# Retention, a softplus feed-forward layer and top-1 experts on one core: loading the first three chunks at once

## The chip, the cores and the metric

The kernel runs on one core of a Trainium2 chip. Its engines work side by side and meet only at semaphores: TensorE multiplies matrices, VectorE and ScalarE work element by element, GpSimd does the same more slowly, and SyncE issues the DMAs (each engine issues its own instructions strictly in order). The metric is the time of one execution on the device in microseconds (us), lower is better.

## The reference

What has to be computed, cut to what matters (4 batches, 8 heads, 768 positions, head size 64; all inputs and outputs are float32):

```python
# stage 1: decayed linear attention, one state per batch and head
for t in range(S):
    state = gamma * state + einsum('bhd,bhe->bhde', k[:, :, t], v[:, :, t])
    y[:, :, t] = scale * einsum('bhd,bhde->bhe', q[:, :, t], state)
x = y.transpose(0, 2, 1, 3).reshape(3072, 512)
# stage 2: dense feed-forward, 512 -> 2048 -> 512
h = x @ w_in
x = (maximum(h, 0) + log1p(exp(-abs(h)))) @ w_out          # softplus
# stage 3: each token goes through the one of 8 experts that its gate picks, 512 -> 1024 -> 512
e = argmax(x @ w_gate, axis=1)
out = softmax_weight_of_e * (maximum(x @ w1[e], 0) @ w2[e])
```

## The kernel before, in words

**Stage 1 by chunks.** The recurrence is cut into chunks of 128 positions, six for each batch. A chunk needs four loads of 256 KB: kT, qT, k and v. `heads` (TensorE, L1156) makes the scores of the eight heads from kT and qT; `masked` (VectorE, L724, twice) multiplies them by the table `decay` into two buffers of probabilities; on GpSimd, `decays` multiplies q by `qdec` (L449) and k by `kdec` (L451); `attend_to` (TensorE) adds up the values under the probabilities (L1171), updates the running state in PSUM (L1178) and, from the second chunk on, adds the part that comes from the state before (L1184). The state that it reads is made by `read_state` (VectorE, L731). The chunk's result goes to `XS` as a rounded high part (`x_high`, ScalarE, L547) and the rest as a low part (`x_low`, VectorE, L739), because stage 2 multiplies in a format that keeps fewer bits: three products (high·high, high·low, low·high) stand for one.

**Stage 2 by blocks and strips.** Three chunks make a block of 384 tokens; there are eight blocks. A block runs through 16 strips of the 2048 hidden columns. `strip_h` (TensorE, L1205, 12 matmuls) makes a strip of h; ScalarE computes the softplus in three passes (L578, L580, L582) and rounds it (`strip_high`, L562); VectorE finishes it (`strip`, L763) and takes the low part (`strip_low`, L767); `strip_out` (TensorE, L1220, 9 matmuls) multiplies it by w_out. TensorE runs `strip_h(g)` two strips ahead of `strip_out(g - 2)`. The attention of the next block is laid between the strips: in the turn of g = 2, 7 and 12 the `heads` of one chunk stands right behind `strip_h(g)` (list `A1_AT`), and `attend_to` in the turns 4, 9 and 14 (`A2_AT`). In the first block these are chunks 3, 4 and 5.

**The dense weights.** w_in and w_out (4 MB each) come in eight pieces of 1 MB, w_in and w_out in turn, through three staging buffers `raw[0..2]`. Each piece is rounded into `W` by `piece_high` (ScalarE, L552), and `piece_low` (VectorE, L745) writes the low part and so frees the staging buffer. Pieces 0, 1 and 2 are split while the first three chunks are computed, pieces 3 to 7 during the first block, in the strips that `PIECES_AT` lists. `strip_h(g)` needs piece 2(g/4), `strip_out(g)` piece 2(g/4) + 1, for g = 0, 4, 8 and 12.

**The queue of loads.** All these loads are issued by SyncE in one written order, and it waits, in order, until the buffer of each is free. In the first block the order is: chunk 3, pieces 3 to 7, the small `gate_k`, chunk 4, `w_gate` (2 MB, its buffer lies where the staging was, so it waits until the last piece is split), chunk 5. A chunk has one set of load buffers, so chunk c + 1 is loaded when chunk c has left them.

**The start.** `load_chunk(0, 0)` brings chunk 0 and the tables (`decay` 512 KB, `qdec` 256 KB, the small table 164.5 KB), and then for each chunk its loads and one piece follow each other. TensorE goes through `heads` and `attend_to` chunk by chunk, in PSUM banks given by `START_AT`. Nothing of stage 2 can start before x_low of chunk 2.

Stage 3 (routing, gathers, expert weights) is not touched.

Of the kernel before, what the change touches and what calls it, by code (L numbers as in the profile page):

```python
# [68 lines left out]
PIECES_AT = [1, 3, 4, 6, 7]  # L69
# [34 lines left out]
def build(nc, qT, kT, k, v, w_in, w_out, w_gate, w_gate_k, w1, w2, table, out):  # L104
    x_rows = nc.dram_tensor("x_rows", [NTOK, D], F32, kind="Internal").ap()

    with ExitStack() as ctx:
# [223 lines left out]
        def _(sp):  # L331
            def load_chunk(b, c6):
                c = b * CB + c6
                first = isinstance(c, int) and c == 0
                src = slice(c6 * D, (c6 + 1) * D)
                if not first:
                    sp.wait_ge(s_qk if isinstance(c, int) and c <= SUB else s_att, c)
                sp.dma_start(kT_c, kT[b_at(b), :, src].rearrange("o p n -> (o p) n")).then_inc(s_kT, 16)
                if not first:
                    sp.wait_ge(s_qd, c)  # L340
                sp.dma_start(qT_c, qT[b_at(b), :, src].rearrange("o p n -> (o p) n")).then_inc(s_qT, 16)
                if first:
# [26 lines left out]
            load_chunk(0, 3)  # L369
            for n in range(3, 2 * NPIECE):  # L370
                load_piece(n)
# [33 lines left out]
            def one(i, half, attend, first):  # L405
# [5 lines left out]
                if first:  # L411
                    sp.wait_ge(s_wlo, 2 * NPIECE)
# [30 lines left out]
        def _(pool):  # L443
            def decays(b, c6):
                c = b * CB + c6
                pool.wait_ge(s_qT, 16 * (c + 1))
                if not (isinstance(c, int) and c == 0):
                    pool.wait_ge(s_att, c)
                pool.tensor_tensor(qd, qT_c, qdec, ALU.mult).then_inc(s_qd, 1)  # L449
                pool.wait_ge(s_k, 16 * (c + 1))  # L450
                pool.tensor_tensor(blk(k_c, H), blk(k_c, H), kdec[:, c6, :].unsqueeze(2).broadcast_to([P, H, HD]),  # L451
                                   ALU.mult).then_inc(s_kd, 1)

            pool.wait_ge(s_tab, 32)
            for c6 in range(SUB):
                decays(0, c6)
# [83 lines left out]
        def _(act):  # L540
# [8 lines left out]
            def piece_high(n):  # L549
                act.wait_ge(s_raw[n % 3], 16 * (n // 3 + 1))  # L550
# [3 lines left out]
            for c6 in range(SUB):  # L554
                x_high(0, c6, START_AT[c6])
                piece_high(c6)
# [41 lines left out]
            def shifted(i, half, attend, first=False):  # L598

                m = 2 * i + half  # L600
                for g in range(1, GF + 1):
# [4 lines left out]
                    if first and g in PIECES_AT:  # L606
                        piece_high(3 + PIECES_AT.index(g))
# [106 lines left out]
        def _(dve):  # L714
# [27 lines left out]
            def piece_low(n):  # L742
                dve.wait_ge(s_whi, n + 1)
# [3 lines left out]

            for c6 in range(SUB):
# [196 lines left out]
            def shifted(i, half, attend, first):  # L945
                m = 2 * i + half
                for g in range(1, GF + 1):
# [8 lines left out]
                    if first and g in PIECES_AT:  # L956
                        piece_low(3 + PIECES_AT.index(g))
# [186 lines left out]
        def _(pe):  # L1144
            def heads(b, c6, at=0):
# [3 lines left out]
                pe.wait_ge(s_kT, 16 * (c + 1))  # L1149
                pe.wait_ge(s_qT, 16 * (c + 1))  # L1150
                if at == 0 and not (isinstance(c, int) and c == 0):
                    pe.wait_ge(s_xlo, 1 if isinstance(c, int) and c < SUB else c)
                for h in range(H):
                    rows = slice((h % 2) * HD, (h % 2 + 1) * HD)
                    cols = slice((h // 2) * P, (h // 2 + 1) * P)
                    last = pe.matmul(ps[:, at + h % 2, cols], kT_c[rows, cols], qT_c[rows, cols],  # L1156
                                     start=True, stop=True)
                last.then_inc(s_qk, 1)

            def attend_to(b, c6, at=0):  # L1160
                c = b * CB + c6
                pe.wait_ge(s_v, 16 * (c + 1))
# [6 lines left out]
                for h in (0, 2, 1, 3, 4, 6, 5, 7):  # L1169
                    bank, out_rows, out_cols = spot(h)  # L1170
                    last = pe.matmul(ps[out_rows, at + bank, out_cols], v_c[:, h * HD:(h + 1) * HD],  # L1171
                                     probs_of(h % 2, c)[:, (h // 2) * P:(h // 2 + 1) * P], start=(h < 4),
                                     stop=True, skip_group_check=True)
                if c6 < CB - 1:
                    for h in range(H):
                        rows = slice((h % 2) * HD, (h % 2 + 1) * HD)
                        head = slice(h * HD, (h + 1) * HD)
                        last = pe.matmul(blk(ps_s, PAIRS)[rows, h // 2, :], k_c[:, head], v_c[:, head],  # L1178
                                         start=(c6 == 0 and h < 2), stop=True, skip_group_check=True)
                if c6:  # L1180
                    for h in range(H):
# [277 lines left out]
```

## Time and profile before

| quantity | value |
|---|---|
| runs | 1039.24, 1039.69, 1042.95 us; median 1039.69 us |
| profiled execution | 1037.87 us, span 1036.1 us |
| mean granted TensorE clock | 0.987 of full speed |
| TensorE busy | 993.4 us, 96% of the span |
| VectorE / ScalarE / GpSimd busy | 507.7 / 430.3 / 164.3 us (49%, 42%, 16%) |
| chain that ended last | TensorE 90%, VectorE 2%, DMA 2%, "issue" 2%, ScalarE 1%, GpSimd 1% |

How to read it: the span runs from the first to the last instruction of the profile; the profiled execution's own time is 1.8 us longer. TensorE is busy in nine tenths or more of each slice except the first and the last; in the first of the 40 slices (26 us each) it is busy for four tenths and in the second for seven. The page and the answers of the trace name an instruction by its line in the kernel and by the tensors that it writes and reads; `arena` is the big shared buffer in which most small tiles lie. "SPq" rows are DMA issues of SyncE. Rows of L1171, L1156, L1178 and L1184 count two records for each matmul.

### The profile page before, as it was taken

The page shows a single profiled execution, that of the slowest core. Times are in us where ns is not written, and L with a number is a line of the kernel's source. Part 1 is how long each engine was busy: PE and PEld are TensorE (multiplying, and loading weights), DVE is VectorE, ACT ScalarE, POOL GpSimd, SP SyncE. Part 2 cuts the span into 40 slices and gives each one's busy share as a digit, 9 for nine tenths or more (in the row PEclk, how much of TensorE's full clock was granted, in tenths as well). Part 3 has the DMA queues.
Part 4 walks back from the last instruction along what each step waited for, and adds up shares of the span by engine and source line. Part 5 has one row for each costly group of instructions (what it writes and reads, how often), then busy time and mean ns, then how long its engine had stood idle before and what let it go on. Part 6 is the DMA issues. An engine that isn't in the chain of part 4 may idle for free.

```text
span 1036.1 us, 18904 instructions
## 1 busy us (share of the span) xinstructions
PE 993.4 (96%) x5968; PEld 859.0 (83%) x5969; DVE 507.7 (49%) x997; ACT 430.3 (42%) x754; POOL 164.3 (16%) x172
## 2 busy tenths in 40 slices
PE   4799999999999999999999999999999999999994
PEld 4688888888788888888888898787888888888783
DVE  2563265455465465456456487555222422445552
ACT  1473543533443443444444546424223323435451
POOL 2200010111111111111111000221111312232230
PEclk8799999999999999999999999999999999999998
DMA  6633121121121121121121013237111311552570
GB/s 220 251 105 114 41 72 42 41 72 42 43 71 42 41 72 41 43 71 42 41 72 41 31 41 122 73 122 274 53 40 40 114 40 40 193 205 73 189 261 15
DMA packets 28631, 91.89 MB, mean 89 GB/s; under 512 B 4046, under 2 KB 4174, under 8 KB 23312
## 3 DMA queue, kind: packets, MB, share of 16 engines
q1 hardware_dynamic: 23760, 76.48, 21.2%
q0 software_dynamic: 4800, 14.42, 4.3%
q8 instruction: 50, 0.82, 0.3%
q14 instruction: 21, 0.17, 0.1%
HBM read 78.30 MB, written 13.89 MB: 89 GB/s over the span
## 4 chain that ended last, share of the span: by engine, by line
PE 90%; DVE 2%; issue 2%; DMA 2%; ACT 1%; DVEq 1%; POOL 1%; ACTq 0%; SPq 0%; POOLq 0%
PE ps L1205 25%; PE ps L1220 25%; PE ps L1334 15%; PE ps L1309 14%; PE ps L1171 3%; PE ps L1156 2%; PE ps L1319 2%; PE ps L1184 1%; PE ps L1293 1%; PE ps L1178 1%; POOL arena L451 1%; DMA arena<-k 1%; DMA small_tab<-table 1%; DVE W L987 1%; DMA arena<-x_rows,arena 1%
## 5 line engine op out<-in xcount | busy, mean ns | idle before, releaser
L1205 PE MATMUL ps<-XS,W 128*128 128x384 f32 x1536 | 292.0, 338 | 4.8 <-issue 2.2
L1220 PE MATMUL ps<-W,GS 128*128 128x512 f32 x1152 | 292.1, 398 | 2.2 <-DVE GS L767 2.2
L1205 PEld LDWEIGHTS ps<-XS,W 128*128 128x128 f32 x1536 | 273.6, 189 | 17.6 <-issue 2.8
L1220 PEld LDWEIGHTS ps<-W,GS 128*128 128x128 f32 x1152 | 211.3, 188 | 48.4 <-DVE GS L767 3.3
L1334 PE MATMUL ps<-W,XS 128*128 (+1 forms) x696 | 167.3, 396 | 4.5 <-DVE XS L997 4.5
L1309 PE MATMUL ps<-W,XS 128*128 (+1 forms) x696 | 170.6, 394 | 0.0
L578 ACT ACTIVATE arena<-ps 128x384 f32<-128x384 f32 x128 | 62.8, 491 | 232.1 <-PE ps L1205 228.6
L1334 PEld LDWEIGHTS ps<-W,XS 128*128 128x128 f32 x696 | 129.7, 190 | 31.6 <-issue 5.6
L1309 PEld LDWEIGHTS ps<-W,XS 128*128 128x128 f32 x696 | 128.4, 188 | 25.5 <-DVE XS L991 0.3
L763 DVE SCALAR_TENSOR_TENSOR arena<-ps,arena 128x384 f32<-128x384 f32 x128 | 71.1, 555 | 135.0 <-ACT arena L582 135.0
L778 DVE CUSTOM_DVE_ANT_0 arena<-arena 128x512 bf16<-128x512 f32 x168 | 128.3, 802 | 0.0
L449 POOL TENSOR_TENSOR arena<-arena 128x512 f32<-128x512 f32 x24 | 37.6, 1567 | 465.9 <-DMA arena<-qT 445.4
L649 ACT ACTIVATE XS<-ps 128x512 fp32r<-128x512 f32 x58 | 31.5, 595 | 171.3 <-PE ps L1319 155.4
L767 DVE TENSOR_TENSOR GS<-arena,GS 128x384 fp32r<-128x384 f32 x128 | 75.0, 586 | 0.1
L997 DVE TENSOR_TENSOR XS<-ps,XS 128x512 fp32r<-128x512 f32 x58 | 37.4, 686 | 76.4 <-ACT XS L649 41.9
L582 ACT ACTIVATE arena<-arena 128x384 f32<-128x384 f32 x128 | 67.2, 525 | 4.0
L580 ACT ACTIVATE arena<-arena 128x384 f32<-128x384 f32 x128 | 67.2, 525 | 4.0
L987 DVE TENSOR_TENSOR W<-arena,W 128x2048 f32 (+1 forms) x28 | 62.8, 2286 | 9.6 <-ACT W L630 9.6
L739 DVE TENSOR_TENSOR XS<-ps,XS 128x512 fp32r<-128x512 f32 x24 | 16.6, 692 | 100.6 <-ACT XS L547 100.6
L562 ACT ACTIVATE GS<-arena 128x384 fp32r<-128x384 f32 x128 | 65.0, 508 | 0.5 <-DVE arena L763 0.5
L547 ACT ACTIVATE XS<-ps 128x512 fp32r<-128x512 f32 x24 | 14.4, 598 | 113.1 <-PE ps L1184 89.7
L1004 DVE TENSOR_SCALAR arena<-ps,arena 128x512 f32<-128x512 f32 x28 | 20.9, 748 | 81.5 <-PE ps L1334 81.5
(160 smaller groups left out, 675.7 us busy)
## 6 DMA issues: line engine op xcount, KB each, us to landing
arena<-w SPq DMA_DIRECT2D x32, 1024.0 KB, 7.0
arena<-kT SPq DMA_DIRECT2D x24, 256.0 KB, 2.7
arena<-qT SPq DMA_DIRECT2D x24, 256.0 KB, 2.9
arena<-v SPq DMA_DIRECT2D x24, 256.0 KB, 4.1
arena<-k SPq DMA_DIRECT2D x24, 256.0 KB, 4.2
x_rows<-arena SPq DMA_DIRECT2D x24, 256.0 KB, 4.5
arena<-w_in SPq DMA_DIRECT2D x4, 1024.0 KB, 6.8
arena<-w_out SPq DMA_DIRECT2D x4, 1024.0 KB, 7.7
```

The source lines that it names most:

```text
L562: act.activation(GS[:, par, 0, :], soft[par], ACT.Copy).then_inc(s_ghi, 1)
L578: act.activation(soft[par], ps_h[par], ACT.Abs).then_inc(s_abs, 1)
L580: act.activation(soft[par], soft[par], ACT.Exp, scale=-1.0).then_inc(s_exp, 1)
L582: act.activation(soft[par], soft[par], ACT.Ln, bias=1.0).then_inc(s_ln, 1)
L763: dve.scalar_tensor_tensor(soft[par], ps_h[par], 0.0, soft[par], ALU.max, ALU.add).then_inc(s_g, 1)
L767: dve.tensor_tensor(GS[:, par, 1, :], soft[par], GS[:, par, 0, :].bitcast(F32), ALU.subtract).then_inc(s_glo, 1)
L778: dve.tensor_tensor_reduce(out=junk[e % 2], in0=x_out[s], in1=gate_w[:, e * D:(e + 1) * D], scale=1.0, scalar=0.0, op0=ALU.mult, op1=ALU.a ...
L987: dve.tensor_tensor(dst, raw_w[:, cols], hi, ALU.subtract).then_inc(s_out, 1)
L1205: last = pe.matmul(ps_h[g % 2], w_in_s[a][:, g // 4, k_, (g % 4) * P:(g % 4 + 1) * P], xs[half][b][:, k_, :], start=(k_ == 0 and a + b == ...
L1220: last = pe.matmul(ps_x[s], GS[:, g % 2, a, s * P:(s + 1) * P], w_out_s[b][:, g, :], start=(g == 0 and a + b == 0), stop=(g == GF - 1 and ...
L1309: last = pe.matmul(ps_h1[n], tx[a][:, k_ * P:(k_ + 1) * P], w, start=(k_ == 0 and a + b == 0), stop=(k_ == KD - 1 and a == 1))
L1334: last = pe.matmul(ps_y2, th[a][:, k_ * P:(k_ + 1) * P], w, start=(k_ == 0 and a + b == 0), stop=(k_ == GE - 1 and a == 1))
```

## The change

- The first three chunks have buffers of their own: chunk 0 those of before, chunks 1 and 2 four quarters each of `raw[1]` and `raw[2]`. Their loads are issued without a wait, chunk after chunk (`load_first`), with `qdec` moved behind the first two loads of chunk 1. Chunk 3 is issued behind them and behind piece 0.
- Each load has a semaphore that is waited for where its data is used. GpSimd no longer decays q of chunk 0 (nothing reads it), and decays k before q; q of chunk 2 goes to a buffer of its own.
- TensorE issues `heads` of chunk 1 ahead of the attention of chunk 0, and waits for the decayed k only ahead of the state update (`first_attend`). VectorE reads the state after the masks, and takes x_low of a chunk one chunk later.
- Piece 0 comes and is split in two halves. Since `raw[1]` and `raw[2]` hold chunks, pieces 1 and 2 are loaded when chunks 1 and 2 are done. Before the first strip, pieces 0 and 1 are split; pieces 2 to 7 are split in strips 1, 3, 5, 7, 9 and 11 of the first block. Before, pieces 3 to 7 were split in strips 1, 3, 4, 6 and 7.
- `low_done(n)` is the count that says that piece n is split, now with one more for the halves.

```diff
-PIECES_AT = [1, 3, 4, 6, 7]
+PIECES_AT = [1, 3, 5, 7, 9, 11]
...
+        s_qdec = sem("q_decay_loaded")
         s_kT, s_qT, s_k, s_v = sem("kT_loaded"), sem("qT_loaded"), sem("k_loaded"), sem("v_loaded")
         s_raw = [sem(f"raw_loaded{i}") for i in range(3)]
+        s_raw0 = [sem(f"first_raw_half{i}") for i in range(2)]
+        s_qk_in, s_kv_in = ([sem(f"{w}_loaded{c}") for c in (1, 2)] for w in ("qT_kT", "k_v"))
...
+        def loaded(c):
+            return 16 * (c - 1)
+        def chunk(c, i):
+            return raw[c][:, i * D:(i + 1) * D] if isinstance(c, int) and 0 < c < SUB else (kT_c, qT_c, k_c, v_c)[i]
+        def qd_of(c):
+            return start_odd if isinstance(c, int) and c == SUB - 1 else qd
         def probs_of(half, c):
-            return probs_even if half == 0 else start_odd if isinstance(c, int) and c < SUB else kT_c
+            return probs_even if half == 0 else start_odd if isinstance(c, int) and c == 0 else chunk(c, 0)
+        def low_done(n):
+            return n + 2
...
+            def load_first(c):
+                src, rows = slice(c * D, (c + 1) * D), slice(c * P, (c + 1) * P)
+                sp.dma_start(chunk(c, 0), kT[0, :, src]).then_inc(s_qk_in[c - 1] if c else s_kT, 16)
+                sp.dma_start(chunk(c, 1), qT[0, :, src]).then_inc(s_qk_in[c - 1] if c else s_qT, 16)
+                if c == 0:
+                    sp.dma_start(decay, table[:, T_DECAY:T_QDEC]).then_inc(s_dec, 16)
+                if c == 1:
+                    sp.dma_start(qdec, table[:, T_QDEC:T_KDEC]).then_inc(s_qdec, 16)
+                sp.dma_start(chunk(c, 3), v[0, rows, :]).then_inc(s_kv_in[c - 1] if c else s_v, 16)
+                if c == 0:
+                    sp.dma_start(small_tab[:], table[:, T_KDEC:T_COLS]).then_inc(s_tab, 16)
+                sp.dma_start(chunk(c, 2), k[0, rows, :]).then_inc(s_kv_in[c - 1] if c else s_k, 16)
             def load_chunk(b, c6):
                 c = b * CB + c6
-                first = isinstance(c, int) and c == 0
                 src = slice(c6 * D, (c6 + 1) * D)
-                if not first:
-                    sp.wait_ge(s_qk if isinstance(c, int) and c <= SUB else s_att, c)
+                sp.wait_ge(s_qk if isinstance(c, int) and c == SUB else s_att, 1 if isinstance(c, int) and c == SUB else c)
                 sp.dma_start(kT_c, kT[b_at(b), :, src].rearrange("o p n -> (o p) n")).then_inc(s_kT, 16)
-                if not first:
+                if not (isinstance(c, int) and c == SUB):
                     sp.wait_ge(s_qd, c)
                 sp.dma_start(qT_c, qT[b_at(b), :, src].rearrange("o p n -> (o p) n")).then_inc(s_qT, 16)
-                if first:
-                    sp.dma_start(decay, table[:, T_DECAY:T_QDEC]).then_inc(s_dec, 16)
+                if isinstance(c, int) and c == SUB:
+                    sp.wait_ge(s_att, 1)
                 else:
                     sp.wait_ge(s_att, c)
                     sp.wait_ge(s_kd, c)
                 rows = slice(c6 * P, (c6 + 1) * P)
                 sp.dma_start(v_c, v[b_at(b), rows, :].rearrange("o p n -> (o p) n")).then_inc(s_v, 16)
-                if first:
-                    sp.dma_start(qdec, table[:, T_QDEC:T_KDEC]).then_inc(s_tab, 16)
-                    sp.dma_start(small_tab[:], table[:, T_KDEC:T_COLS]).then_inc(s_tab, 16)
                 sp.dma_start(k_c, k[b_at(b), rows, :].rearrange("o p n -> (o p) n")).then_inc(s_k, 16)
             def b_at(b):
                 return bass.ds(b, 1)
             def load_piece(n):
-                if n >= 3:
-                    sp.wait_ge(s_wlo, n - 2)
+                if n < 3:
+                    sp.wait_ge(s_att, n + 1)
+                else:
+                    sp.wait_ge(s_wlo, low_done(n - 3))
                 src = w_in if n % 2 == 0 else w_out
                 sp.dma_start(raw[n % 3], src[:, (n // 2) * PIECE:(n // 2 + 1) * PIECE]).then_inc(s_raw[n % 3], 16)
-            load_chunk(0, 0)
-            load_piece(0)
-            load_chunk(0, 1)
-            load_piece(1)
-            load_chunk(0, 2)
-            load_piece(2)
-            load_chunk(0, 3)
-            for n in range(3, 2 * NPIECE):
+            for c in range(SUB):
+                load_first(c)
+            for i in range(2):
+                cols = slice(i * PIECE // 2, (i + 1) * PIECE // 2)
+                sp.dma_start(raw[0][:, cols], w_in[:, cols]).then_inc(s_raw0[i], 16)
+            load_chunk(0, SUB)
+            for n in range(1, 2 * NPIECE):
...
-                    sp.wait_ge(s_wlo, 2 * NPIECE)
+                    sp.wait_ge(s_wlo, low_done(2 * NPIECE - 1))
...
+            pool.wait_ge(s_tab, 16)
+            pool.wait_ge(s_k, 16)
+            decay_k(0, 0)
+            pool.sem_inc(s_qd, 1)
+            pool.wait_ge(s_qdec, 16)
+            for c in range(1, SUB):
+                pool.wait_ge(s_kv_in[c - 1], 32)
+                decay_k(c, c)
+                pool.wait_ge(s_qk_in[c - 1], 32)
+                if c == SUB - 1:
+                    pool.wait_ge(s_att, 1)
+                pool.tensor_tensor(qd_of(c), chunk(c, 1), qdec, ALU.mult).then_inc(s_qd, 1)
...
+            def first_piece_high(i):
+                act.wait_ge(s_raw0[i], 16)
+                cols = slice(i * PIECE // 2, (i + 1) * PIECE // 2)
+                act.activation(W[:, 0, 0, cols], raw[0][:, cols], ACT.Copy).then_inc(s_whi, 1)
+            x_high(0, 0, START_AT[0])
+            x_high(0, 1, START_AT[1])
+            first_piece_high(0)
+            first_piece_high(1)
+            x_high(0, 2, START_AT[2])
+            piece_high(1)
...
-                        piece_high(3 + PIECES_AT.index(g))
+                        piece_high(2 + PIECES_AT.index(g))
...
             for c6 in range(SUB):
                 if c6 == 1:
-                    dve.wait_ge(s_tab, 32)
-                if c6:
-                    read_state(0, c6)
+                    dve.wait_ge(s_tab, 16)
                 masked(0, c6, 0, START_AT[c6])
                 masked(0, c6, 1, START_AT[c6])
                 if c6:
-                    piece_low(c6 - 1)
-                x_low(0, c6, START_AT[c6])
-            piece_low(SUB - 1)
+                    read_state(0, c6)
+                    x_low(0, c6 - 1, START_AT[c6 - 1])
+            first_piece_low(0)
+            first_piece_low(1)
+            x_low(0, SUB - 1, START_AT[SUB - 1])
+            piece_low(1)
...
-                        piece_low(3 + PIECES_AT.index(g))
+                        piece_low(2 + PIECES_AT.index(g))
...
+            def first_attend(c, at):
+                if c:
+                    pe.wait_ge(s_kv_in[c - 1], 32)
+                else:
+                    pe.wait_ge(s_v, 16)
+                pe.wait_ge(s_probs, 2 * c + 2)
+                values(c, at)
+                pe.wait_ge(s_kd, c + 1)
+                if c:
+                    pe.wait_ge(s_state, c)
+                    pe.wait_ge(s_qd, c + 1)
+                last = update(c, c)
+                if c:
+                    last = from_state(c, at)
+                last.then_inc(s_att, 1)
+            heads(0, 0, START_AT[0])
+            heads(0, 1, START_AT[1])
+            first_attend(0, START_AT[0])
+            first_attend(1, START_AT[1])
+            heads(0, 2, START_AT[2])
+            first_attend(2, START_AT[2])
...
-                    pe.wait_ge(s_wlo, 2 * (g // 4) + 1)
+                    pe.wait_ge(s_wlo, low_done(2 * (g // 4)) if g else 1)
...
+                    if isinstance(n, int) and n == 0 and k_ == KD // 2:
+                        pe.wait_ge(s_wlo, 2)
```

TensorE at the start of the program, before. L1156 is `heads`, L1171 the values, L1178 the state update, L1184 the part from the state.

```order
L1156 MATMUL ps<-arena 128x128 [waits qT_loaded,kT_loaded]
L1156 MATMUL ps<-arena 128x128 x7
L1171 MATMUL ps<-arena 64x128 [waits probs_ready,k_decayed,v_loaded]
L1171 MATMUL ps<-arena 64x128 x7
L1178 MATMUL ps<-arena 64x64 x8
L1156 MATMUL ps<-arena 128x128 [waits qT_loaded,kT_loaded]
L1156 MATMUL ps<-arena 128x128 x7
L1171 MATMUL ps<-arena 64x128 [waits k_decayed,state_ready,probs_ready,q_decayed,v_loaded]
```

The same place in the changed kernel, where these are L1214, L1222, L1231 and L1239.

```order
L1214 MATMUL ps<-arena 128x128 [waits qT_loaded,kT_loaded]
L1214 MATMUL ps<-arena 128x128 x7
L1214 MATMUL ps<-arena 128x128 [waits qT_kT_loaded1]
L1214 MATMUL ps<-arena 128x128 x7
L1222 MATMUL ps<-arena 64x128 [waits probs_ready,v_loaded]
L1222 MATMUL ps<-arena 64x128 x7
L1231 MATMUL ps<-arena 64x64 [waits k_decayed]
L1231 MATMUL ps<-arena 64x64 x7
L1222 MATMUL ps<-arena 64x128 [waits probs_ready,k_v_loaded1]
L1222 MATMUL ps<-arena 64x128 x7
L1231 MATMUL ps<-arena 64x64 [waits q_decayed,state_ready,k_decayed]
```

The second chunk's scores now stand ahead of the first chunk's values, and the values no longer wait for the decayed k.

VectorE at the last piece of the dense weights, before: L745 is `piece_low(7)`, in strip 7. The mask behind it (L724) is the second one of chunk 4.

```order
L731 TENSOR_TENSOR arena<-ps,small_tab 128x256 [waits attention_done]
L724 TENSOR_TENSOR arena<-ps,arena 128x512 [waits attention_done,scores_ready]
L763 SCALAR_TENSOR_TENSOR arena<-ps,arena 128x384 [waits ln_done]
L767 TENSOR_TENSOR GS<-arena,GS 128x384 [waits softplus_high]
L745 TENSOR_TENSOR W<-arena,W 128x2048 [waits dense_high]
L724 TENSOR_TENSOR arena<-ps,arena 128x512 [waits attention_done,scores_ready]
```

The last piece in the changed kernel: L793 is `piece_low(7)`, in strip 11. L818 and L822 are a strip's two operations, L779 and L772 behind it the state and the first mask of chunk 5.

```order
L818 SCALAR_TENSOR_TENSOR arena<-ps,arena 128x384 [waits ln_done]
L822 TENSOR_TENSOR GS<-arena,GS 128x384 [waits softplus_high]
L793 TENSOR_TENSOR W<-arena,W 128x2048 [waits dense_high]
L779 TENSOR_TENSOR arena<-ps,small_tab 128x256 [waits attention_done]
L772 TENSOR_TENSOR arena<-ps,arena 128x512 [waits attention_done,scores_ready]
```

The last split moved from between the two masks of chunk 4 to right ahead of the masks of chunk 5.

SyncE in the first block of the changed kernel: the last piece, `gate_k`, chunk 4 (L368 to L379), `w_gate`, and chunk 5's first loads. The order before is the same.

```order
L390 DMA arena<-w_out 128x2048 [waits dense_low]
L400 DMA gate_k<-w_gate_k 128x32
L368 DMA arena<-kT 128x512 [waits attention_done]
L371 DMA arena<-qT 128x512 [waits q_decayed]
L378 DMA arena<-v 128x512 [waits k_decayed,attention_done]
L379 DMA arena<-k 128x512
L441 DMA arena<-w_gate 128x4096 [waits dense_low]
L368 DMA arena<-kT 128x512 [waits attention_done]
L371 DMA arena<-qT 128x512 [waits q_decayed]
```

No row moved here; piece 7 still waits for piece 4's split and `w_gate` for piece 7's, and these splits stand in other strips now.

## Rows read from the trace of the kernel before

**Rows 1.** Chain of waits, first 60 us; start, length (us), what ran or was awaited.
```profile
3.09 6.08 DMA small_tab<-table
...
14.83 3.03 DMA arena<-k
...
17.92 2.73 POOL arena L451
...
20.90 1.98 PE ps L1171 x16
...
23.73 1.11 PE ps L1184 x16
...
36.54 3.82 PE ps L1205 x12
...
54.95 1.02 PE ps L1171 x16
```

**Rows 2.** Chain of waits from 36 us to 130 us, one warm strip.
```profile
83.80 2.10 PE ps L1205 x12
```

**Rows 3.** Busy time by windows; last three columns granted clock, DMA share, GB/s.
```profile
8.00:10.00 2.00, 0.00 (x0) 0.00 (x0) 0.77 (x2) 0.00 (x0) 0.76 (x1) 1.00 0.99 407
```

**Rows 4.** Timeline of all engines, one early chunk; start, length, what, idle before.
```profile
24.73 1.79 PE L1156 MATMUL ps<-arena 64*128 64x128 f32 x16
24.86 0.60 ACT L547 ACTIVATE XS<-ps 128x512 fp32r<-128x512 f32 x1 [8.00 <-PE ps L1184]
...
25.36 1.90 ACT L552 ACTIVATE W<-arena 128x2048 fp32r<-128x2048 f32 x1
25.49 0.69 DVE L739 TENSOR_TENSOR XS<-ps,XS 128x512 fp32r<-128x512 f32 x1 [5.75 <-ACT XS L547]
...
26.10 0.41 DVE L731 TENSOR_TENSOR arena<-ps,small_tab 128x256 f32<-128x256 f32 x1
...
26.56 1.29 DVE L724 TENSOR_TENSOR arena<-ps,arena 128x512 f32<-128x512 f32 x2
...
27.77 2.28 DVE L745 TENSOR_TENSOR W<-arena,W 128x2048 fp32r<-128x2048 f32 x1
```

**Rows 5.** Busy time by windows again, granted clock third from last.
```profile
26.00:26.50 0.50, 0.50 (x8) 0.32 (x6) 0.50 (x2) 0.50 (x1) 0.26 (x1) 0.92 0.45 53
...
29.50:30.00 0.50, 0.00 (x0) 0.00 (x0) 0.50 (x1) 0.00 (x0) 0.50 (x1) 0.50 1.00 410
...
39.50:40.00 0.50, 0.50 (x3) 0.50 (x3) 0.39 (x1) 0.00 (x0) 0.50 (x1) 0.77 0.65 262
```

**Rows 6.** Timeline around piece 7 and chunk 4 in the first block.
```profile
56.74 0.33 SPq L361 DMA_DIRECT2D arena<-w_out  x1
...
58.07 0.43 SPq L341 DMA_DIRECT2D arena<-qT  x1
...
62.96 0.51 ACT L562 ACTIVATE GS<-arena 128x384 fp32r<-128x384 f32 x1
...
69.72 1.16 PE L1156 MATMUL ps<-arena 64*128 64x128 f32 x16
```

**Rows 7.** DMA issues in 58.05 to 58.4 us: KB, us to landing.
```profile
arena<-qT SPq DMA_DIRECT2D x1, 256.0 KB, 6.1
```

**Rows 8.** Timeline around w_gate and chunk 5.
```profile
76.01 0.33 SPq L413 DMA_DIRECT2D arena<-w_gate  x1
...
81.97 0.42 SPq L341 DMA_DIRECT2D arena<-qT  x1
...
91.64 0.51 ACT L562 ACTIVATE GS<-arena 128x384 fp32r<-128x384 f32 x1
...
94.21 1.16 PE L1156 MATMUL ps<-arena 64*128 64x128 f32 x16
```

**Rows 9.** DMA issues at 76.01 and 81.97 us: KB, us to landing.
```profile
arena<-w_gate SPq DMA_DIRECT2D x1, 2048.0 KB, 8.1
...
arena<-qT SPq DMA_DIRECT2D x1, 256.0 KB, 3.5
```

More of the change, by code:

```diff
@@ L443, in _, with decay_k @@
         def _(pool):
+            def decay_k(c, c6):
+                pool.tensor_tensor(blk(chunk(c, 2), H), blk(chunk(c, 2), H),
+                                   kdec[:, c6, :].unsqueeze(2).broadcast_to([P, H, HD]), ALU.mult).then_inc(s_kd, 1)
             def decays(b, c6):
                 c = b * CB + c6
-                pool.wait_ge(s_qT, 16 * (c + 1))
-                if not (isinstance(c, int) and c == 0):
-                    pool.wait_ge(s_att, c)
+                pool.wait_ge(s_qT, loaded(c))
+                pool.wait_ge(s_att, c)
                 pool.tensor_tensor(qd, qT_c, qdec, ALU.mult).then_inc(s_qd, 1)
[L450 to L456, printed above, removed]
+                pool.wait_ge(s_k, loaded(c))
+                decay_k(c, c6)
+            pool.wait_ge(s_tab, 16)
[10 more added lines that the diff above has]
+                pool.tensor_tensor(qd_of(c), chunk(c, 1), qdec, ALU.mult).then_inc(s_qd, 1)
             def one(i, half, attend, first):
@@ L742, in piece_low @@
             def piece_low(n):
-                dve.wait_ge(s_whi, n + 1)
+                dve.wait_ge(s_whi, low_done(n))
                 cols = slice((n // 2) * PIECE, (n // 2 + 1) * PIECE)
@@ L1155, in heads, with values, update, from_state @@
                     cols = slice((h // 2) * P, (h // 2 + 1) * P)
-                    last = pe.matmul(ps[:, at + h % 2, cols], kT_c[rows, cols], qT_c[rows, cols],
+                    last = pe.matmul(ps[:, at + h % 2, cols], chunk(c, 0)[rows, cols], chunk(c, 1)[rows, cols],
                                      start=True, stop=True)
                 last.then_inc(s_qk, 1)
+            def values(c, at):
+                v_in, halves = chunk(c, 3), [probs_of(half, c) for half in range(2)]
+                for h in (0, 2, 1, 3, 4, 6, 5, 7):
+                    bank, out_rows, out_cols = spot(h)
+                    last = pe.matmul(ps[out_rows, at + bank, out_cols], v_in[:, h * HD:(h + 1) * HD],
+                                     halves[h % 2][:, (h // 2) * P:(h // 2 + 1) * P], start=(h < 4),
+                                     stop=True, skip_group_check=True)
+                return last
+            def update(c, c6):
+                for h in range(H):
+                    rows = slice((h % 2) * HD, (h % 2 + 1) * HD)
+                    head = slice(h * HD, (h + 1) * HD)
+                    last = pe.matmul(blk(ps_s, PAIRS)[rows, h // 2, :], chunk(c, 2)[:, head], chunk(c, 3)[:, head],
+                                     start=(c6 == 0 and h < 2), stop=True, skip_group_check=True)
+                return last
+            def from_state(c, at):
+                for h in range(H):
+                    bank, out_rows, out_cols = spot(h)
+                    rows = slice((h % 2) * HD, (h % 2 + 1) * HD)
+                    last = pe.matmul(ps[out_rows, at + bank, out_cols], blk(state, PAIRS)[rows, h // 2, :],
+                                     blk(qd_of(c), PAIRS)[rows, h // 2, :], start=False, stop=True,
+                                     skip_group_check=True)
+                return last
             def attend_to(b, c6, at=0):
                 c = b * CB + c6
-                pe.wait_ge(s_v, 16 * (c + 1))
+                pe.wait_ge(s_v, loaded(c))
                 if c6:
@@ L1168, in attend_to @@
                 pe.wait_ge(s_probs, 2 * c + 2)
[L1169 to L1173, printed above, removed]
-                if c6 < CB - 1:
[L1175 to L1179, printed above, removed]
@@ L1180, in attend_to @@
-                if c6:
-                    for h in range(H):
-                        bank, out_rows, out_cols = spot(h)
-                        rows = slice((h % 2) * HD, (h % 2 + 1) * HD)
-                        last = pe.matmul(ps[out_rows, at + bank, out_cols], blk(state, PAIRS)[rows, h // 2, :],
-                                         blk(qd, PAIRS)[rows, h // 2, :], start=False, stop=True,
-                                         skip_group_check=True)
-                last.then_inc(s_att, 1)
@@ L1189, in _ @@
-            for c6 in range(SUB):
-                heads(0, c6, START_AT[c6])
-                attend_to(0, c6, START_AT[c6])
+                last = values(c, at)
+                if c6 < CB - 1:
+                    last = update(c, c6)
+                if c6:
+                    last = from_state(c, at)
+                last.then_inc(s_att, 1)
+            def first_attend(c, at):
+                if c:
+                    pe.wait_ge(s_kv_in[c - 1], 32)
+                else:
+                    pe.wait_ge(s_v, 16)
[7 more added lines that the diff above has]
+                if c:
+                    last = from_state(c, at)
+                last.then_inc(s_att, 1)
```

17 lines of the change are left out of this document (10 added, 7 removed).

## The prediction

> **What bounds the kernel now.** I read the page's slices first: TensorE is busy nine tenths or more everywhere but at the two ends, so only the first 40 us or so can be shortened, and anything later that makes TensorE wait is paid in full. Next the chain of waits of the first 60 us [rows 1]. It shows the start as a ladder: k of chunk 1 is issued when chunk 0 is done and travels 3.03 us, GpSimd decays it for 2.73 us, and only then TensorE multiplies (1.98 us for the values, up to 1.11 us for the part from the state). The first strip starts at 36.54 us. Then the windows for the clock [rows 3, 5], and the timeline of the loads in the first block [rows 6, 8] with their landings [rows 7, 9], because the change also moves the splits of the weight pieces, on which SyncE's queue hangs.
>
> **Part 1, the start (gain).** The first six loads still bring 1700 KB, as the first six did that ended with the small table, so k of chunk 0 lands when that did: 3.09 + 6.08 = 9.2 us [rows 1]. Then kT and qT of chunk 1, 0.52 MB, at the 407 GB/s of [rows 3]: 1.3 us, landing at 10.5. From there by durations of [rows 1, 4]:
> - scores of chunk 1, 1.79: 12.3. These now stand ahead of chunk 0's attention: that is the price of the new order. Values 1.98 and update 0.85 (22.88 to 23.73) of chunk 0: 15.1.
> - chunk 1: masks 1.29, values 1.98, update 0.85, part from the state 1.11: 20.4. Its k (3.0 MB into the queue) lands near 12.5 and its decay takes at most 2.73, well before 18.4. The ladder's k wait and decay are gone.
> - chunk 2: scores 1.79, masks 1.29: 23.5.
>
> From here the clock decides. With the slow clock: values, update and state part 3.94, x_high 0.60, x_low 0.69: first strip at 28.8, a gain of 7.7. With the fast clock the attention takes about half (1.02 against 1.98 for the values [rows 1]), 2.05, and x_high ends at 26.2; but then VectorE is late: after the masks it has read_state 0.41, x_low of chunk 1 0.69, two half pieces of 2.28 together, x_low of chunk 2 0.69, which ends at 27.6. ScalarE has the half pieces ready (chunk 1 done at 20.4, x_high 0.60, 1.90 for both: 22.9), and the halves have landed: 5.15 MB into the queue are some 18 us even at the 300 to 400 GB/s seen. So the strips start 8.9 us earlier, and the first of them runs in 2.10 instead of 3.82 us [rows 1, 2], another 1.7: 10.6 together.
>
> Which clock? The granted clock rose to 1.0 (2.4 GHz) at about 26.1 us, after 5.2 us of work that began at 20.9, fell to 0.5 (1.2 GHz) at 29.5, 3.0 us after TensorE stopped at 26.5, and rose again at 39.7, 3.2 us after the strips began [rows 1, 4, 5]. In the changed kernel TensorE works from 16.4 to 22.2 us without a gap and its two gaps are 1.3 us, shorter than the 3.0 us that the clock survived. I take the fast clock. The Trainium skill, "TensorE: Matmul & The Clock Gate", section "HAM oscillation — how this bites in real kernels", says the same of bursts between DMA waits, that long waits make every burst start cold and that keeping the work together keeps the engine warm. By it the gain is 10.6; the trace agrees on the fall and the rise but has no 1.3 us gap at the fast clock.
>
> Other edits of the start cost nothing: GpSimd does one product less, and the SyncE issues (0.33 to 0.43 us each, 18 in a row, 8 us) run ahead of the data they bring. Pieces 1 and 2 are now loaded after chunks 1 and 2 (20.4 and about 26): piece 1 is split before the first strips are needed by strip_out, and piece 2 is due 8 us after the strips begin.
>
> **Part 2, the loads of chunks 4 and 5 (loss).** The splits moved from strips 1, 3, 4, 6, 7 to 1, 3, 5, 7, 9, 11, with one piece more behind the first strip. Piece 7's load waits until piece 4 is split, and chunk 4 is issued behind it on SyncE. I keep the clock of the profile before, in which TensorE runs without gaps from 42.6 us, and ask when each event comes in it.
> - Before, piece 4 was split in strip 3 and piece 7 issued at 56.74; qT of chunk 4 landed at 58.07 + 6.1 = 64.2 [rows 6, 7], 7.4 after it, and its scores began at 69.72: 5.5 us of slack.
> - Now it is split in strip 5. ScalarE's rounding of the strip ends there at 63.5 [rows 6]; piece_high 1.90, piece_low 2.28 [rows 4]: piece 7 is issued at 67.7, and qT of chunk 4 lands 7.4 later, at 75.1. TensorE wants it at 69.7, in order, with strip_out(5) behind it: **a wait of 5.4 us**.
> - `w_gate` waits for piece 7's split, which moved from strip 7 to 11: ScalarE ends there at 92.15 [rows 8], plus 1.90 and 2.28: `w_gate` at 96.4 instead of 76.01. Chunk 5 is issued behind it. The 2 MB land after 8.1 us, at 104.5; before, qT of chunk 5 landed 1.4 us after w_gate did (85.5 against 84.1, though issued 6 us later [rows 8, 9]). So 105.9, wanted at 94.2: **a wait of 11.7 us**. Behind piece 7 the tail was 2.5 us rather than 1.4, so up to 12.8.
> - Both waits are longer than the 3.0 us that the clock survived. A restart at the slow clock costs 1.7 us where it lasts 3.2 us (3.82 against 2.10) and some 2.8 where it lasts 5.2. I take 2.0 each, 4.0 in all; between 0 and 5.6.
>
> On the queue the Trainium skill, "DMA: Bandwidth & Descriptors", section "Queues, rings and completion order", says that each DMA engine takes the descriptors of a ring in order, so that chunk 5 can't pass w_gate. The trace only shows qT landing 3.5 us after its issue while the end of w_gate was still under way; by the rule the wait is 11.7, without it that of the third rival below.
>
> **Sum**: −10.6 + 5.4 + 11.7 + 4.0 = +10.5 us. The profiled execution of before took 1037.87, so 1048.4; the median is 1.8 above that execution, so 1050.2 against 1039.69. Everything after the first block is as before, since TensorE sets the pace there.
>
> **Rivals.**
> 1. The start stays at the slow clock: gain 7.7 and not 10.6. For it: the burst from 11.6 to 16.2 us ran at slow durations all through. Time 1053.1. Chance 0.20.
> 2. Faster: the loads of chunks 4 and 5 are hidden anyway, and only the start counts: 1029.1. It needs chunk 4 issued before about 62.3 in the old clock and w_gate before 82.7; for it would speak a piece split earlier than its strip. The written order of ScalarE and VectorE doesn't allow that. Chance 0.05.
> 3. Chunk 5's loads are served beside w_gate, and qT lands 3.5 us after its issue at 97.3, as at 81.97 [rows 9]: the wait is 6.6, the time 1045.1. Against it: then nearly all of w_gate had been moved. Chance 0.10.
> 4. The clock holds through the waits: 1046.2. Against it the falls at 29.5 after 3.0 us. Chance 0.07.
> 5. The early loads come slower than the 407 GB/s, with 18 loads outstanding, and chunk 0 waits behind chunk 1's scores: 3 to 5 us less gain, 1054. Chance 0.08.
>
> My forecast has the remaining 0.50. About 0.5% (5 us) is what a measurement can tell from no change. Below 1034.5 only rival 2 lies: faster 0.05. Between 1034.5 and 1044.9 lie the low ends of rivals 3 and 4: same 0.07. Slower 0.88. The range takes in rivals 1 and 3 to 5: 1045 to 1055.
>
> **What would show it.** In the profile after: first strip near 27.6 (28.8 with the slow clock) instead of 36.5, with the granted clock at 1.0 from some 22 us on. TensorE's list of waits: scores waiting for DMA of qT (or kT) twice in the first block, near 5.4 and 11.7 us, the first some 33 us after the first strip, the second some 63 us after it. Slices 3 and 4 of the clock row under full. The waits of ScalarE and VectorE grow by the same amounts. The forecast is wrong if TensorE has no gap there; then the reading of SyncE's queue is at fault. If the gaps are there but the first strip is not before 32 us, part 1 is.

## The result and the profile after

The changed kernel takes 1047.68 us (median of 4 runs, 1047.15 to 1051.2), the kernel before 1039.99 us (1039.24 to 1042.95). The ratio is 1.0076, 95% interval 1.0046 to 1.0105: about 8 us slower. The forecast was 1050.2 us, 1045 to 1055.

TensorE's list of waits in the first 130 us of the changed kernel (what waited, for what: us in all, times, the longest):

```profile
PE ps L1214 <- DMA arena<-kT: 11.2, 1, 11.2
PE ps L1214 <- DMA arena<-qT: 8.4, 2, 4.5
PE ps L1214 <- issue: 4.5, 1, 4.5
PE ps L1222 <- DVE arena L772: 3.1, 2, 1.6
```

L1214 is `heads`. The two waits for qT are those of the start; the one of 11.2 us for kT and the one of 4.5 us under "issue" are the new ones, at chunks 5 and 4. That the second is booked as "issue" need not mislead: the timeline has the decay of q, which waits for the same qT, start 0.02 us before it.

The chain of waits over the start of the changed kernel (start, length, what), to hold against [rows 1]:

```profile
4.04 6.41 DMA arena<-qT
...
10.49 2.08 PE ps L1214 x13
12.57 1.91 PE ps L1222 x16
...
16.91 1.09 PE ps L1222 x16
18.00 0.46 PE ps L1231 x16
18.47 0.60 PE ps L1239 x16
19.07 1.12 PE ps L1214 x16
...
22.42 2.27 DVE W L800 x2
24.69 0.61 DVE XS L787
25.30 0.04 issue
25.34 2.39 PE ps L1298 x12
```

The ladder of k and its decay is gone. The first strip starts at 25.34 us instead of 36.54, and its 12 matmuls take 2.39 instead of 3.82 us. Values of chunk 0 take 1.91 us, those of chunk 1 1.09: the clock has risen between them. The last thing ahead of the strips is VectorE, with the half pieces and x_low.

The timeline around chunk 4 and chunk 5 (start, length, what, idle before), which answers to [rows 6] and [rows 8]:

```profile
52.68 2.29 DVE L793 TENSOR_TENSOR W<-arena,W 128x2048 fp32r<-128x2048 f32 x1 [1.20 <-ACT W L591]
...
55.00 0.33 SPq L390 DMA_DIRECT2D arena<-w_out  x1
...
56.33 0.43 SPq L371 DMA_DIRECT2D arena<-qT  x1
...
61.65 2.08 PE L1214 MATMUL ps<-arena 64*128 64x128 f32 x16 [4.49 <-issue]
...
63.66 3.68 PE L1313 MATMUL ps<-W,GS 128*128 128x512 f32 x9
```

```profile
88.18 2.29 DVE L793 TENSOR_TENSOR W<-arena,W 128x2048 fp32r<-128x2048 f32 x1 [1.20 <-ACT W L591]
...
90.50 0.33 SPq L441 DMA_DIRECT2D arena<-w_gate  x1
...
91.47 0.42 SPq L371 DMA_DIRECT2D arena<-qT  x1
...
99.70 2.08 PE L1214 MATMUL ps<-arena 64*128 64x128 f32 x16 [11.22 <-DMA arena<-kT]
...
101.71 3.46 PE L1313 MATMUL ps<-W,GS 128*128 128x512 f32 x9
```

Each time a split ends, SyncE issues the big load within 0.1 us, chunk 4 or 5 behind it, and TensorE stands still until qT is there. The scores then take 2.08 us instead of 1.16 and the strip_out 3.68 and 3.46 instead of 2.3: the slow clock (the granted clock reads 0.50, the level of 1.2 GHz, from 60.0 to 66.5 us and from 90.5 to 104 us). The DMA landings say how long the queue took (KB, us from issue to landing; w_gate, then chunk 5's qT):

```profile
arena<-w_gate SPq DMA_DIRECT2D x1, 2048.0 KB, 7.8
```

```profile
arena<-qT SPq DMA_DIRECT2D x1, 256.0 KB, 8.1
```

w_gate lands at 98.3 us and qT at 99.6, 1.3 behind it.

The account, by where the scores of each chunk start (before, after, difference): chunk 3 at 44.94 and 32.32, −12.6; chunk 4 at 69.72 and 61.65, so +4.5 for the wait; chunk 4's attention at 79.38 and 73.57, +2.3 slow clock; chunk 5 at 94.21 and 99.70, +11.3; the first scores of the next block at 122.42 and 129.94, +2.0. Sum +7.5, and it stays: at 536.71 and 544.24 us the difference is 7.5 again. The two profiled executions differ by 9.5 (1037.87 and 1047.34); the other 2 arise behind that point and are within what varies from run to run. From the last scores that I follow (146.32 before, 153.83 after, and their like) to the end of the span it took 889.8 us before, 891.7 after, and between 888.9 and 894.8 in the eleven experiments. Totals of single profiles thus differ by some us for reasons that have nothing to do with the first block.

### The profile page after: what moved, and what is told of

Read it like the earlier page. It is cut to its first block, busy times and chain, and to the rows that moved or that the text cites. A ratio compares the mean times of both kernels' runs of the same rounds, so it can differ in the third digit from the quotient of the medians.

```text
span 1045.5 us, 18902 instructions
## 1 busy us (share of the span) xinstructions
PE 993.3 (95%) x5968; PEld 858.7 (82%) x5969; DVE 505.4 (48%) x998; ACT 430.6 (41%) x755; POOL 157.6 (15%) x171
## 4 chain that ended last, share of the span: by engine, by line
PE 88%; DMA 3%; DVE 3%; issue 2%; ACT 2%; DVEq 1%; SPq 0%; ACTq 0%; POOL 0%; POOLq 0%
PE ps L1313 25%; PE ps L1298 24%; PE ps L1427 14%; PE ps L1402 14%; PE ps L1214 3%; PE ps L1222 2%; PE ps L1412 2%; DMA arena<-kT 1%; PE ps L1239 1%; PE ps L1386 1%; PE ps L1231 1%; DMA arena<-w 1%; DMA arena<-qT 1%; ACT W L678 1%; DVE W L1042 1%
## 5 line engine op out<-in xcount | busy, mean ns | idle before, releaser
L818 DVE SCALAR_TENSOR_TENSOR arena<-ps,arena 128x384 f32<-128x384 f32 x128 | 71.1, 555 | 136.3 <-ACT arena L630 136.3
L480 POOL TENSOR_TENSOR arena<-arena 128x512 f32<-128x512 f32 x21 | 31.3, 1489 | 476.7 <-DMA arena<-qT 470.3
L1052 DVE TENSOR_TENSOR XS<-ps,XS 128x512 fp32r<-128x512 f32 x58 | 37.5, 686 | 78.5 <-ACT XS L697 43.7
L822 DVE TENSOR_TENSOR GS<-arena,GS 128x384 fp32r<-128x384 f32 x128 | 74.1, 579 | 0.1
L772 DVE TENSOR_TENSOR arena<-ps,arena 128x512 f32<-128x512 f32 x48 | 32.7, 687 | 81.7 <-PE ps L1214 67.6
```

The source lines that it names most:

```text
L818: dve.scalar_tensor_tensor(soft[par], ps_h[par], 0.0, soft[par], ALU.max, ALU.add).then_inc(s_g, 1)
L822: dve.tensor_tensor(GS[:, par, 1, :], soft[par], GS[:, par, 0, :].bitcast(F32), ALU.subtract).then_inc(s_glo, 1)
```

## The experiments

Two theories had to be told apart: the late splits hold SyncE's queue, and with it chunks 4 and 5; or the loss comes from something else in the new arrangement. Times are medians; ratios are to the kernel before on the same chip, with 95% intervals. The changed kernel's ratio for comparison: 1.0076.

**1. Early splits.** In the changed kernel:

```diff
-PIECES_AT = [1, 3, 5, 7, 9, 11]
+PIECES_AT = [1, 2, 3, 4, 6, 7]
```

> The changed kernel with one list altered: pieces 2 to 7 are split in strips 1, 2, 3, 4, 6, 7 instead of 1, 3, 5, 7, 9, 11, so that the last four stand where they stood in the kernel before. Theory (the late splits hold SyncE's queue, and chunks 4 and 5 behind it): both waits of TensorE (4.5 and 11.3 us) and the slow clock after each (2.3 and 2.0 us) go, 20.1 us less than the changed kernel: the start's gain of 12.6 us alone is left, about 1027.4 us. Rival (the waits come from somewhere else, such as loads that are slower because they are closer together): one of the two waits stays, 1033 us or more.

Measured 1027.95 us, ratio 0.9866 (0.9839 to 0.9893). TensorE's waits for loads are those of the start alone:

```profile
PE ps L1214 <- DMA arena<-qT: 8.8, 2, 4.4
PE ps L1222 <- DVE arena L772: 3.1, 2, 1.6
PE ps L1298 <- DVE XS L787: 1.5, 1, 1.5
PE ps L1298 <- DVE arena L818: 0.2, 1, 0.2
```

One list turned 0.8% slower into 1.3% faster.

**2. Late splits, chunks ahead in the queue.** The splits stay in strips 1 to 11, but SyncE issues chunk 4 ahead of piece 7 and chunk 5 ahead of w_gate:

```diff
             for n in range(1, 2 * NPIECE):
+                if n == 2 * NPIECE - 1:
+                    load_chunk(0, SUB + 1)
                 load_piece(n)
...
                     if not first:
                         load_chunk(b, c0)
-                    load_chunk(b, c0 + 1)
+                        load_chunk(b, c0 + 1)
                 if first:
+                    load_chunk(b, c0 + 2)
                     sp.wait_ge(s_wlo, low_done(2 * NPIECE - 1))
...
                 if attend:
-                    load_chunk(b, c0 + 2)
+                    if not first:
+                        load_chunk(b, c0 + 2)
```

> The changed kernel with the late splits kept, but in SyncE's order chunk 4 is issued ahead of piece 7 and chunk 5 ahead of w_gate. Theory (it is the place in the queue, not the work of the splits): as the run with early splits, 1027.4 us, no wait of TensorE for kT or qT after the start. Rival (the late splits themselves make ScalarE or VectorE late in strips 5 to 11): the waits stay in part, with VectorE or ScalarE as their end, more than 1030 us.

Measured 1028.23 us, ratio 0.9867 (0.9840 to 0.9894), the same as with early splits. Its trace has chunk 4 issued at 44.3 us and w_gate at 83.6, after chunk 5, and TensorE waits for no load behind the start. From the scores of chunk 3 to those of chunk 5 it took 49.6 us, with early splits 49.3. So the late splits as such cost at most some tenths of a microsecond; the loss comes from what waits behind them on SyncE.

**3. The kernel before with late splits.** Neither the early loads nor the new order:

```diff
-PIECES_AT = [1, 3, 4, 6, 7]
+PIECES_AT = [3, 5, 7, 9, 11]
```

> The kernel before, with nothing changed but the splits of pieces 3 to 7, which stand in strips 3, 5, 7, 9, 11 instead of 1, 3, 4, 6, 7. Theory: the loss alone, without the gain at the start. Waits of 5.4 and 11.7 us as worked out in the prediction and about 2.1 us of slow clock after each: 1040 + 21.3 = 1061 us. Rival (the waits need the early start, since it moves the strips closer to the loads): under 1050 us.

Measured 1060.69 us, ratio 1.0182 (1.0155 to 1.0208): the loss alone, 18.9 us by the ratio where 21.3 were expected. Two waits of TensorE, 4.81 and 11.26 us; the list books both for kT (the row of 15.4 us is the start's, as in the kernel before):

```profile
PE ps L1156 <- DMA arena<-kT: 16.1, 2, 11.3
PE ps L1171 <- POOL arena L451: 15.4, 3, 5.3
```

The loss does not need the early start. Waits and restarts were both expected about 1 us too high: from the scores of chunk 3 to the first scores of the next block this kernel took 96.6 us and the kernel before 77.5, which is 19.1 more. The waits are 16.1 of it (17.1 expected), and the two restarts are left with 3.1 together (4.2 expected).

**4 and 5. One chunk ahead at a time.** The two halves of the edit of experiment 2, each alone.

> The changed kernel, with only chunk 4 issued ahead of piece 7; chunk 5 stays behind w_gate. Theory: only the first wait goes, 4.5 us and 2.3 us of slow clock after it: 6.8 us less than the changed kernel, 1040.9 us where the changed kernel stands at 1047.7; the second wait stays at 11.2 us. Rival (the waits are linked: with the first gone, the second grows by as much, since w_gate is issued at a fixed time): 1045 to 1048 us and a second wait of 15 us or more.

> The changed kernel, with only chunk 5 issued ahead of w_gate; chunk 4 stays behind piece 7. Theory: the second wait goes, 11.2 us and 2.0 us of slow clock: 13.2 us less, 1034.5 us where the changed kernel stands at 1047.7. The first wait stays at 4.5 us. Rival (chunk 5's own loads, or those of w_gate beside the strips, take a good part of the wait anyway): 1038 us or more.

Chunk 4 ahead: 1040.99 us, ratio 1.0006 (0.9993 to 1.0020), 0.7% under the changed kernel; the second wait stays at 11.23 us. Chunk 5 ahead: 1035.21 us, ratio 0.9946 (0.9929 to 0.9964), 1.3% under it; the first wait stays, at 4.94 us. The scores of chunk 5 in the one, those of chunk 4 in the other:

```profile
94.76 2.08 PE L1216 MATMUL ps<-arena 64*128 64x128 f32 x16 [11.23 <-DMA arena<-kT]
```

```profile
62.36 2.08 PE L1216 MATMUL ps<-arena 64*128 64x128 f32 x16 [4.94 <-DMA arena<-kT]
```

By ratios 7.3 and 13.5 us: together 20.8, against the 21.7 us between 1.0076 and 0.9867. The two waits are independent.

**6. Waits at the start again.** Early splits, with the loads of chunks 1 and 2 held until the chunk before has moved on:

```diff
+                if c:
+                    sp.wait_ge(s_qk, c)
                 sp.dma_start(chunk(c, 0), kT[0, :, src])...
...
+                if c:
+                    sp.wait_ge(s_att, c)
                 sp.dma_start(chunk(c, 3), v[0, rows, :])...
```

> As the run with early splits, but SyncE waits again before it loads the next of the first three chunks: kT and qT when the scores of the chunk before are done, v and k when its attention is done. Buffers and order stay. Theory (the start's gain comes from the loads issued at once): v and k of chunk 1 and 2 land 3 us after the attention before, and k's decay stands behind them, so each of the two chunks ends 3 to 4 us later, the piece 0 halves too: 1034 to 1037 us instead of 1027.9. Rival (the gain comes from the new order of TensorE and from x_low and the splits out of the way): 1029 us or less.

Measured 1038.57 us, ratio 0.9982 (0.9970 to 0.9994). The rival, that the gain comes from the new order alone, falls: without the immediate loads nearly all of the 13 us are gone. Whether the immediate loads would bring them without the new order was not tried. The time is 1.6 us more than the range that was expected. The timeline shows the size that I had missed: the values of chunk 1 come at 18.99 us after a wait for k, and at the slow clock, and so do those of chunk 2.

```profile
18.99 1.98 PE L1226 MATMUL ps<-arena 128*64 128x128 f32 x16 [3.27 <-DMA arena<-k]
...
27.19 1.98 PE L1226 MATMUL ps<-arena 128*64 128x128 f32 x16 [1.51 <-DMA arena<-k]
...
33.79 4.44 PE L1302 MATMUL ps<-XS,W 128*128 128x384 f32 x15 [2.38 <-DVE XS L791]
```

The loads issued at once pay twice: no wait for k, and a clock that rises earlier. The scores of chunk 2 took 2.08 us here; in the changed kernel and the seven experiments that keep its start they took 1.16.

**7. A filler in the long wait.** In the changed kernel, ahead of the scores of chunk 5, matmuls whose result is overwritten:

```diff
+                        if first and a == A1_AT[2]:
+                            pe.wait_ge(s_xlo, SUB + 2)
+                            for _ in range(80):
+                                pe.matmul(ps[:, 0, 0:256], w_in_s[0][:, 0, 0, 0:P], xs[0][0][:, 0, 0:256],
+                                          start=True, stop=True, skip_group_check=True)
                         if a in A1_AT:
```

> The changed kernel with 80 matmuls of 128x256, whose result is overwritten, put ahead of the scores of chunk 5, where TensorE waits 11.2 us. They last some 9.6 us. Theory (TensorE restarts at 1.2 GHz because it stood still): the scores of chunk 5 take 1.16 instead of 2.08 us and the strip_out behind them 2.3 instead of 3.46 us; 2.0 us less than the changed kernel, 1045.7 us where that stands at 1047.7. Rival (the slow stretch has another cause, such as the DMA traffic or a limit on power): the same slow durations, and no change or a loss.

Measured 1046.18 us, ratio 1.0050 (1.0034 to 1.0067), but the scores took 2.08 us still: the expected durations did not come. In the timeline (start, length, what, idle before) the filler ends 2.58 us before kT's wait does:

```profile
88.67 9.75 PE L1447 MATMUL ps<-XS,W 128*128 128x256 f32 x80
101.00 2.08 PE L1214 MATMUL ps<-arena 64*128 64x128 f32 x16 [2.58 <-DMA arena<-kT]
103.01 2.92 PE L1313 MATMUL ps<-W,GS 128*128 128x512 f32 x9
```

The slow stretch came later and was shorter (the strip_out at 2.92 instead of 3.46), which speaks for the theory, but the test was not clean. So again with 98 of them.

> As the run with 80 filler matmuls, with 98 of them, some 11.9 us, so that TensorE stands still for about half a microsecond instead of 2.6 ahead of the scores of chunk 5. Theory (standing still is what brings the clock down, and 2.6 us were enough for it): scores 1.16 us instead of 2.08, strip_out 2.3 instead of 2.92, the granted clock 1.0 all through 88 to 108 us, about 1045.5 us. Rival (the slow stretch comes from something else than TensorE standing still): scores at 2.08 us again.

```profile
88.64 11.91 PE L1447 MATMUL ps<-XS,W 128*128 128x256 f32 x98
100.71 1.16 PE L1214 MATMUL ps<-arena 64*128 64x128 f32 x16 [0.16 <-issue]
101.80 2.34 PE L1313 MATMUL ps<-W,GS 128*128 128x512 f32 x9
```

The granted clock in three windows of this run (third number from the right), and of the changed kernel in the same windows:

```profile
94.00:98.00 4.00, 4.00 (x36) 4.00 (x35) 0.00 (x0) 0.00 (x0) 0.00 (x0) 1.00 0.96 401
98.00:100.00 2.00, 2.00 (x19) 2.00 (x18) 0.00 (x0) 0.00 (x0) 0.00 (x0) 1.00 1.04 400
100.00:104.00 4.00, 3.84 (x31) 3.16 (x30) 2.09 (x4) 0.00 (x0) 2.29 (x2) 1.00 0.11 41
```

```profile
94.00:98.00 4.00, 0.00 (x0) 0.00 (x0) 0.00 (x0) 0.00 (x0) 0.00 (x0) 0.50 0.94 395
98.00:100.00 2.00, 0.30 (x2) 0.34 (x4) 0.00 (x0) 0.00 (x0) 0.33 (x1) 0.50 1.00 381
100.00:104.00 4.00, 4.00 (x21) 3.30 (x20) 2.19 (x4) 0.00 (x0) 1.98 (x2) 0.50 0.02 9
```

Measured 1044.66 us, ratio 1.0043 (1.0025 to 1.0060), 3.4 us under the changed kernel by ratio, where about 2 were expected; the interval takes those in. The traces give the size better. From the scores of chunk 5 to the first scores of the next block it took 28.21 us here (100.71 to 128.92), the same as in the kernel before (94.21 to 122.42), and 30.24 in the changed kernel (99.70 to 129.94): the slow clock costs 2.0 us. Since the scores started 1.0 later here, 1.0 us of gain is left in the first block; the rest of the 3.4 is not shown to come from the filler. The DMA traffic is the same in both (about 400 GB/s). It is TensorE's standing still that costs the clock.

**8. Chunk 0's attention first.** Early splits, and one line moved:

```diff
             heads(0, 0, START_AT[0])
-            heads(0, 1, START_AT[1])
             first_attend(0, START_AT[0])
+            heads(0, 1, START_AT[1])
             first_attend(1, START_AT[1])
```

> As the run with early splits, and TensorE does the attention of chunk 0 ahead of the scores of chunk 1 (one line moved). Theory: the scores of chunk 1 wait for data until 10.5 us and hold up chunk 0, whose values could start at 8.7; chunk 0 ends at about 11.5 instead of 15.4, the masks of chunk 1 start at 13.6 instead of 15.5 and the strips up to 1.8 us sooner: 1025.6 to 1026.5 us. Rival (the clock rises later, since TensorE's work is split by gaps in another way): values and scores of chunks 1 and 2 at the slow clock, no gain or a loss of 1 to 3 us, 1027.4 to 1030 us.

Measured 1027.13 us, ratio 0.9856 (0.9828 to 0.9884), 0.8 us less than experiment 1, where 1025.6 to 1026.5 us were expected. Since the two kernels differ by less than their intervals, both were measured again on one chip.

> The kernel with early splits again, beside the next one, with more rounds. 1027.9 us as before (ratio to the kernel before 0.9866).

> The kernel with early splits and chunk 0's attention first, again. In the profile of the first look the scores of chunk 3 and all behind them stood 3.0 to 3.2 us earlier than with the early splits alone, but the time was only 0.8 us less. Theory (the gain is real and the rest of the program varies by some 2 us from run to run): 1.0 to 3.2 us less than with early splits alone. Rival (it was the clock's luck at the start in that one run): no difference, under 0.5 us.

Early splits: 1027.91 us, ratio 0.9882 (0.9857 to 0.9906). Chunk 0 first: 1025.96 us, ratio 0.9864 (0.9836 to 0.9893), the lowest median of the study. In the traces the scores of chunk 2 start at 20.48 and 17.39 us, those of chunk 3 at 33.77 and 30.69; in the first pair it was 32.75 and 29.79. Within each pair it is 3.0 to 3.1 us, but a part of that is where the clock happened to rise: the same start with chunk 1's scores first has those of chunk 3 anywhere from 32.07 to 34.17 us in eight profiles. The 29.79 and 30.69 lie below all of them, so that a gain in the first block is seen, and its size is not settled. In the total, 0.8 and 2.0 us of medians are left with overlapping intervals, so that it shortens the whole isn't shown.

## Why the prediction was right

**The first wait.** Forecast 5.4 us, measured 4.5. The place, the cause and piece 7's issue right behind piece 4's split were as said. The term that was off is the landing: qT of chunk 4 landed 6.5 us after piece 7's issue (55.00 to 56.33 + 5.2) and not 7.4 as in [rows 6, 7]. Piece 7 itself took 4.9 us in both profiles; what shrank is the tail behind it, 2.5 us before and 1.6 after, though the same loads stood in the queue. Why is open. In the four other profiles in which TensorE waited here, the wait was 4.76 to 4.94 us.

**The second wait.** Forecast 11.7, measured 11.2. The tail behind w_gate was 1.3 us against 1.4 from [rows 8, 9]; w_gate itself took 7.8 instead of 8.1. The rival in which chunk 5 is served beside w_gate would have had 6.6: qT took 8.1 us from issue to landing. The Trainium skill, "DMA: Bandwidth & Descriptors", section "Queues, rings and completion order", says that each DMA engine consumes descriptors in ring order; the trace agrees, with chunk 5's qT landing 1.3 us behind w_gate.

**The clock after each wait.** Forecast 2.0 each, measured 2.3 and 2.0. For the second the filler shows that it comes from TensorE's standing still; for the first that is taken over from it. In experiment 3 the two cost 3.1 together, so a restart was worth 1.6 to 2.3 us in these runs. Rival 4 falls.

**The start.** Forecast a gain of 10.6 us with the strips at 27.6, measured 12.6 with the strips at 25.3. The step that was mis-sized is "from here the clock decides", which took the fast clock only from chunk 2 on. In this profile the clock had risen between chunk 0 and chunk 1: the values of chunk 1 took 1.09 us, not 1.98, and the scores of chunk 2 1.16, not 1.79. The other terms held: k of chunk 0 by 9.25 (forecast 9.2), scores of chunk 1 at 10.49 (10.5), chunk 0 done at 15.35 (15.1), VectorE last before the strips, and rival 1 (slow clock) did not come about. How early the clock rises is luck of the run, though. Of the eight profiles with this start, two (experiment 4 and the repeat of experiment 1) have the values of chunk 1 at 1.98 us; their strips start at 27.21 and 26.83 us, close to the forecast's 27.6. The kernel before had a sign of it that the prediction misread: rival 1 says that the burst from 11.6 to 16.2 us ran at slow durations all through, but its scores took 1.85 us and not 2.08, the last matmuls 272 ns where the first took 417. So the clock had risen before the burst ended; in the run of experiment 3 the same scores took 1.23 us.

**The sum.** −12.6 + 4.5 + 11.3 + 4.3 = +7.5, forecast +10.5. The 3 us come from the start (2.0) and the two waits (1.3), less 0.3 of clock. The rival with the waits hidden (2) is out by the two waits themselves and by experiments 1, 3, 4 and 5; that the loads with 18 of them outstanding would be slower (rival 5) is out by the 10.49. One figure of rival 2 is wrong: by the prediction's own terms w_gate was due before 84.7 (94.2 − 8.1 − 1.4), not 82.7. Nothing else hangs on it.

## What to carry to other kernels

A queue that one engine issues in order is a chain of dependences that stands in no data flow: before moving a step that frees a buffer, list what is issued behind the load that waits for it, and when each of those is due. Here a step with no hurry of its own (a weight split) held back two loads: when the queue moved on, TensorE wanted the first 2 us later and had been waiting 2 us for the second. Moving either the step or the place in the queue gave 20 us back. And a wait on TensorE is to be priced with its restart: here about 2 us on top of each.

## What the runs showed of the hardware

In the run with 80 fillers TensorE stood still for 2.58 us (98.42 to 101.00 us), and its scores then ran at the slow durations (2.08 us); the granted clock has a mean of 0.85 from 100.5 to 101.0 us and 0.50 from there. So the clock fell sooner after the stop than in the kernel before, where the prediction read 3.0 us. In the start of the changed kernel gaps of 1.58 and 1.48 us, and in the run with 98 fillers one of 0.16 us, had no slow durations behind them.

In the kernel before the granted clock is given as 1.00 from 0 to 19 us, and in the changed kernel from 0 to 30 us, while matmuls at the beginning run at the slow durations (scores of chunk 0 2.08 us in both kernels, values 1.98 and 1.97 us). So early on the durations tell the level and the granted clock does not; the prediction's sign of a granted clock of 1.0 "from some 22 us on" could not have told it.
